# Tail of a feed-forward layer: turns and logits between half product groups, the first expert's low halves on another engine, gates by their own transfer

## Chip, cores and metric

One Trainium2 chip; the kernel runs on 1 of its cores. The metric is the device time of the kernel in microseconds, the median of three timed runs. A profile of one more execution goes with it.

## The reference

Three layers follow one another, all in float32:

```python
mask = q_bucket[:, :, :, None] == k_bucket[:, :, None, :]
scores = np.where(mask, scale * np.matmul(q, k.transpose(0, 1, 3, 2)), -1e9)
attn = np.exp(scores - np.max(scores, axis=-1, keepdims=True))
x = np.matmul(attn / (np.sum(attn, axis=-1, keepdims=True) + 1e-9), v)   # -> (1536, 512)
...
h = x @ w_in                                   # 512 -> 2048
g = (a[0] + a[1]*h + a[2]*h**2 + a[3]*h**3) / (1 + abs(b[0])*abs(h) + abs(b[1])*h**2 + 1e-6)
x = g @ w_out                                  # 2048 -> 512
...
logits = x @ w_gate                            # 8 experts
expert_idx = np.argmax(logits, axis=1)         # one expert for each token
for e in range(E):                             # w1[e]: 512 x 1024, w2[e]: 1024 x 512
    out[mask] = gate_w[mask, None] * (np.maximum(xe @ w1[e], 0.0) @ w2[e])
```

The first layer is attention over 2 x 8 heads of 768 rows, masked by hash buckets. The change concerns the end of the second layer and the third.

## The kernel before

**Products.** Where full precision is wanted, a factor is split in a high part (rounded to TensorE's float32 format) and a low part (what is left), and three matmuls stand for one: high x high, low x high, high x low. ScalarE makes the high halves (a copy), another engine the low halves (a subtraction).

**Feed-forward.** Sixteen steps of 384 tokens and 512 of the 2048 columns. In each step `up` makes four products of h (banks 0 to 2 of PSUM in turn), ScalarE, VectorE and GpSimd make g of each, and `down(s, t)` multiplies four pieces of g with w_out for the token tile t = 0, 1, 2 (banks 4 to 6, twelve matmuls of 512 columns); VectorE adds the bank to y in `y_add`. `down(s, 1)` and `down(s, 2)` stand two steps later, so that at the end of the loop five remain: step 14 (t = 1, 2) and step 15 (t = 0, 1, 2).

**Tail.** y has twelve tiles of 128 tokens, in four chunks of three. For each tile j `turn_y` transposes y into a bank, ScalarE copies it to yt (`y_turned`, two buffers), `logit` multiplies it with w_gate. For each chunk c VectorE's `choose` finds the expert (oh), `ranks` on TensorE counts the tokens ahead, `place` makes the slot numbers, and GpSimd's `route` writes the three tiles of y, with gate and token number as columns 512 and 513, to their slots in HBM (`routed`) by indirect transfers. The order on each engine is written out by hand; each engine works its own list in order and waits on semaphores.

**Table.** From the totals VectorE works out which expert each of 19 tiles of 128 slots belongs to (`tab_ring`, `tab_need`, `tab_rows`, ...), and then increments `table_done`.

**Experts.** For tile t SyncE loads its rows into xg (`rows_in`, two buffers); TensorE has `turn_x`, `mm1` (24 matmuls), `turn_h`, `mm2` (24 matmuls), VectorE `x_in`, `relu`, `h_in`, `y_out`, GpSimd `scatter`. The weights of expert r lie in a ring of two; each matrix comes in two transfers to one staging area, wraw, which is free again when the low halves are made. ScalarE makes sixteen high halves for each expert (`weights_hi`), GpSimd sixteen low halves (`weights_lo`), in this order with the scatters in between:

```python
            for r in range(1, E):
                weights_lo(0, r, range(8))
                weights_lo(1, r, range(8))
                for t in LATE_SCATTERS[r]:
                    scatter(t)
```

with `LATE_SCATTERS = {1: (), 2: (0, 1), 3: (2,), ...}`. In the data of this case tiles 0, 1 and 2 belong to experts 0, 1 and 2, tiles 3 to 10 to expert 3, tiles 11 to 15 to expert 4, and one tile each to the last three. Line numbers are those of the kernel before unless the text says otherwise: L1336 to L1338 down's matmuls, L1347 turn_y, L1357 logit, L726 GpSimd's low halves, L1156 VectorE's copy of the gates, L1433 turn_x, L1447 to L1449 mm1, L1471 to L1473 mm2.

Of the kernel before, what the change touches and what calls it, by code (L numbers as in the profile page):

```python
# [15 lines left out]
P = 128  # L16
# [3 lines left out]
NTOK, DM, DFF = B * S, H * D, 2048  # L20
# [69 lines left out]
def build(nc, q, k, v, proj, w_in, w_out, a, b, w_gate, w1, w2, consts, out):  # L90
    ctx = ExitStack()
    with ctx:
# [16 lines left out]
        def sem(name):  # L109
            return ctx.enter_context(nc.semaphore(name))  # L110
# [120 lines left out]
        put = Map(late)  # L231
        xg = [put(f"xg{i}", [P, ROW], F32) for i in range(2)]
        xth, xtl = [put(x, [P, KD, P], F32R) for x in ("xth", "xtl")]
# [93 lines left out]
        xt_done = sem("xt_done")  # L327
        gi_done = sem("gi_done")
        hs_done = sem("hs_done")
# [34 lines left out]
        def turn_bank(j):  # L364

            return ps[:, 7 * (j % 2), :]

        def logit_bank(c):

            return 1 if c == NCHUNKS - 1 else c + 1  # L370

# [103 lines left out]
        def _(sp):  # L475
# [121 lines left out]
            for c in range(2):  # L597
                load_weights(sp, 0, 1, c)
# [12 lines left out]

# [3 lines left out]
            for t in range(1, NSLOT_TILES):  # L615
                rows_in(t)
            sp.wait_ge(s_xg[0], 16 * (NSLOT_TILES // 2 + 1))
            sp.wait_ge(s_xg[1], 16 * (NSLOT_TILES // 2))


        @block.gpsimd
        def _(pool):
# [136 lines left out]
        def _(act):  # L759
# [140 lines left out]
            for n in range(NSTEP * M4):  # L900
# [6 lines left out]
                if n % (4 * M4) in PIECE_AT and s // 4 + 1 < NQ:  # L907
                    w_piece(s // 4 + 1, PIECE_AT.index(n % (4 * M4)))
            root(NSTEP * M4 - 1)
            g_hi(act, NSTEP * M4 - 2)  # L910
            g_hi(act, NSTEP * M4 - 1)

            act.wait_ge(h_ready, NSTEP * M4)
            act.wait_ge(s_blank_out, 16 * NROUTED // CT)
            weights_hi(0, 0, range(4))
            for j in range(3):
                y_turned(j)
            exps_of(0)
            weights_hi(0, 0, range(4, 8))
            for j in range(3, 6):  # L920
                y_turned(j)
            exps_of(1)
            for j in range(6, 10):
                y_turned(j)
            exps_of(2)
            for j in range(10, 12):
                y_turned(j)
            exps_of(3)
            weights_hi(1, 0, range(8))
            for c in range(2):  # L930
                load_weights(act, 1, 1, c)

# [17 lines left out]
        def _(dve):  # L950
# [154 lines left out]
            def place(c):  # L1105
# [11 lines left out]
            y_add(NSTEP - 2, 1)  # L1117
            y_add(NSTEP - 2, 2)
            y_add(NSTEP - 1, 0)
            place(0)  # L1120
            choose(1)
            y_add(NSTEP - 1, 1)
            place(1)
            choose(2)
            y_add(NSTEP - 1, 2)
            place(2)
# [3 lines left out]
            dve.wait_ge(total_ready, 1)  # L1130
            link(dve.tensor_tensor(cmp[:, :, :], ps[:, 2, 12 * E:13 * E].unsqueeze(2).broadcast_to([P, E, REGION]),
                                   cst[:, C_MULT:C_MULT + E * REGION].rearrange("p (e i) -> p e i", i=REGION), ALU.is_gt))
# [40 lines left out]
            def y_out(t):  # L1173

                dve.wait_ge(mm2_done, t + 1)
                dve.wait_ge(gi_done, t + 1)
# [16 lines left out]
        def _(pe):  # L1193
# [130 lines left out]

            def down(s, t):
# [7 lines left out]
                for m in range(M4):  # L1333
# [5 lines left out]
                mm.then_inc(y_ready, 1)  # L1339

            def turn_y(j):

                pe.wait_ge(y_added, CT * (NSTEP - NCHUNKS) + j + 1)
                if j >= 2:
                    pe.wait_ge(yt_done, j - 1)
                for kt in range(KD):
                    mm = pe.transpose(turn_bank(j)[:, kt * P:(kt + 1) * P], y[:, j, kt:DM:KD], ident)  # L1347
                mm.then_inc(yt_ready, 1)

            def logit(j):  # L1350

                c, i = j // CT, j % CT
                pe.wait_ge(yt_done, j + 1)
                if c == NCHUNKS - 1:
                    pe.wait_ge(slot_done, 2)
                for kt in range(KD):
# [3 lines left out]
            def logits(c):  # L1360

                j = CT * c
                turn_y(j)
                turn_y(j + 1)
                logit(j)
                turn_y(j + 2)
                logit(j + 1)
                logit(j + 2)

# [32 lines left out]
            logits(1)  # L1402
            down(NSTEP - 1, 1)
            ranks(1)
            logits(2)
            turn_y(9)
            down(NSTEP - 1, 2)
            ranks(2)
            turn_y(10)
            logit(9)  # L1410
            logit(10)
            turn_y(11)
            logit(11)
            ranks(3)
            pe.wait_ge(scum_done, NJ)
            pe.matmul(ps[:, 2, 12 * E:13 * E], cst[:, C_ONE:C_ONE + P], scum[:, NJ, :], start=True, stop=True).then_inc(total_ready, 1)

# [10 lines left out]
            def turn_x(t):  # L1428

                pe.wait_ge(s_xg[t % 2], 16 * (t // 2 + 1))  # L1430
# [78 lines left out]
```

## Time and profile before

| | us |
|---|---|
| median of three timed runs | 913.63 (912.94 to 915.4) |
| profiled execution, its time | 916.21 |
| profiled execution, its span | 914.4 |
| TensorE busy | 810.3 (89%) |
| VectorE, ScalarE, GpSimd busy | 586.3, 489.2, 473.7 |
| mean granted TensorE clock | 0.927 |

The span runs from the first to the last instruction. Busy time of TensorE counts an instruction from its start to its modelled end, at either clock; a granted clock of 1.00 is 2.4 GHz and 0.50 is 1.2 GHz. Idle time is put down to what ended it.

### The profile page before, as it was taken

Reading aid. Unit: us, or ns where it says so; the run is one execution under the profiler, and the core shown is the slowest. Engines: PE = TensorE matmul, PEld = TensorE weight load, DVE = VectorE, ACT = ScalarE, POOL = GpSimd, SP = SyncE. Lnnn points to the kernel's source line nnn. Section 1 sums busy time; section 2 is a strip of 40 time slices with the busy share of each in tenths; the row PEclk is TensorE's granted clock in tenths of the full one; section 3 lists DMA queues with packets and bytes.
Section 4 is the critical chain, followed back from the end, with each engine's and each line's share of the span. In section 5 each row is a group of like instructions: output and inputs, shape, how many; then the busy total and the mean of one; then the engine's idle time right before and its main releaser. Section 6 shows DMA issues by size and latency. Waiting matters only on the chain.

```text
span 914.4 us, 12920 instructions
## 1 busy us (share of the span) xinstructions
PE 810.3 (89%) x4222; PEld 711.2 (78%) x4222; DVE 586.3 (64%) x954; ACT 489.2 (53%) x971; POOL 473.7 (52%) x418
## 2 busy tenths in 40 slices
PE   3699999999998899999999979929659799999965
PEld 2589989998977799989999968827547688888844
DVE  2478888888976788787887772474218545445521
ACT  2478877887897787887886773134412000201230
POOL 1223366335365874674774453479788100541696
PEclk9699999999999899999999997659779799999978
DMA  8597877786626509209600402246554200150322
GB/s 186 126 222 175 195 180 175 179 191 145 187 55 218 198 2 344 95 21 340 218 1 7 178 1 70 104 165 227 195 163 157 96 24 24 38 205 13 117 90 103
DMA packets 69103, 124.12 MB, mean 136 GB/s; under 512 B 30670, under 2 KB 33198, under 8 KB 64944
## 3 DMA queue, kind: packets, MB, share of 16 engines
q1 hardware_dynamic: 61248, 89.34, 35.6%
q10 hardware_dynamic: 5312, 27.66, 9.0%
q0 software_dynamic: 2480, 6.31, 1.8%
q8 instruction: 36, 0.59, 0.3%
q14 instruction: 27, 0.22, 0.1%
HBM read 60.21 MB, written 33.45 MB: 102 GB/s over the span
## 4 chain that ended last, share of the span: by engine, by line
PE 76%; POOL 8%; DVE 7%; ACT 4%; issue 2%; SPq 1%; DMA 1%; ACTq 0%; POOLq 0%
POOL split L726 6%; PE ps L1248 6%; PE ps L1337 5%; PE ps L1336 5%; PE ps L1338 5%; PE ps L1322 4%; PE ps L1320 4%; PE ps L1321 4%; PE ps L1471 4%; PE ps L1447 3%; PE ps L1472 3%; PE ps L1473 3%; PE ps L1239 3%; PE ps L1238 3%; PE ps L1260 3%; PE ps L1449 3%
## 5 line engine op out<-in xcount | busy, mean ns | idle before, releaser
L726 POOL TENSOR_TENSOR split<-wraw,split 128x512 fp32r<-128x512 f32 x128 | 159.2, 1281 | 121.3 <-ACT split L874 121.2
L874 ACT ACTIVATE split<-wraw 128x512 fp32r<-128x512 f32 x128 | 67.9, 616 | 220.4 <-PE ps L1449 126.7
L1016 DVE TENSOR_TENSOR ptl<-ps,pth 128x512 fp32r<-128x512 f32 x144 | 98.8, 686 | 36.1 <-ACT pth L812 34.2
L703 POOL TENSOR_TENSOR hw<-hw,ha 128x384 f32<-128x384 f32 x64 | 65.2, 1019 | 78.1 <-ACT hw L886 78.1
L812 ACT ACTIVATE pth<-ps 128x512 fp32r<-128x512 f32 x144 | 86.7, 602 | 31.6 <-PE ps L1248 31.4
L996 DVE TENSOR_REDUCE negmax<-ps 128x1 f32<-128x768 f32 x96 | 91.1, 949 | 13.9 <-PE ps L1239 13.8
L1447 PE MATMUL ps<-split,xth 128*128 (+1 forms) x152 | 66.1, 435 | 34.3 <-POOL split L726 28.0
L1248 PE MATMUL ps<-cst,pr 128*128 128x128 f32 x576 | 88.1, 273 | 1.6 <-ACT pr L803 1.4
L1320 PE MATMUL ps<-xh,wih 128*128 128x384 f32 x256 | 87.1, 340 | 2.0 <-DVE hp L1050 2.0
L803 ACT ACTIVATE pr<-ps,negmax 128x768 f32<-128x768 f32 x96 | 86.8, 904 | 3.2 <-DVE negmax L996 3.2
L1322 PE MATMUL ps<-xh,wil 128*128 128x384 f32 x256 | 86.8, 339 | 0.0
L1321 PE MATMUL ps<-xl,wih 128*128 128x384 f32 x256 | 86.6, 338 | 0.0
L1336 PE MATMUL ps<-woh,gh 128*128 128x512 f32 x192 | 78.4, 408 | 3.0 <-POOL gl L462 3.0
L1162 DVE TENSOR_SCALAR hs<-ps 128x512 f32<-128x512 f32 x38 | 26.2, 691 | 83.5 <-PE ps L1449 83.5
L462 POOL TENSOR_TENSOR gl<-ha,gh 128x384 fp32r<-128x384 f32 x64 | 65.0, 1015 | 27.2 <-ACT gh L456 27.1
L1337 PE MATMUL ps<-wol,gh 128*128 128x512 f32 x192 | 78.6, 409 | 0.0
L1338 PE MATMUL ps<-woh,gl 128*128 128x512 f32 x192 | 78.1, 407 | 0.0
L1248 PEld LDWEIGHTS ps<-cst,pr 128*128 128x128 f32 x576 | 69.8, 140 | 8.9 <-ACT pr L803 2.5
L1260 PE MATMUL ps<-pth,vs 128*128 128x384 f32 x192 | 74.9, 390 | 2.1 <-DVE ptl L1016 0.9
L1238 PE MATMUL ps<-operand 128*128 128x384 f32 x192 | 70.9, 369 | 5.4 <-DMA operand<-mask 5.4
L1471 PE MATMUL ps<-split,hth 128*128 (+1 forms) x152 | 63.5, 418 | 9.2 <-DVE htl L1171 9.2
L1239 PE MATMUL ps<-operand 128*128 128x384 f32 x192 | 66.1, 344 | 0.0
(160 smaller groups left out, 2028.8 us busy)
## 6 DMA issues: line engine op xcount, KB each, us to landing
wraw<-in_moe_w ACTq DMA_DIRECT2D x26, 1024.0 KB, 5.4
routed<-blank SPq DMA_DIRECT2D x32, 771.0 KB, 14.6
operand<-qk_hi SPq DMA_DIRECT2D x16, 384.0 KB, 4.4
operand<-qk_lo SPq DMA_DIRECT2D x32, 192.0 KB, 4.1
operand<-qk_hi SPq DMA_DIRECT2D x32, 192.0 KB, 4.4
operand<-mask SPq DMA_DIRECT2D x16, 384.0 KB, 4.7
wraw<-in_moe_w SPq DMA_DIRECT2D x6, 1024.0 KB, 6.7
xg<-routed SPq DMA_DIRECT2D x19, 257.0 KB, 2.7
```

What stands on the lines that cost most here:

```text
L726: pool.tensor_tensor(split_piece(E_LO[x], r % 2, k), wraw[:, x, i, :], split_piece(E_HI[x], r % 2, k).bitcast(F32), ALU.subtract).then_inc ...
L1016: dve.tensor_tensor(ptl[:, at:at + CW], ps[:, 4 + c % 2, :], pth[:, at:at + CW].bitcast(F32), ALU.subtract).then_inc(ptl_done, 1)
L1238: pe.matmul(bank, operand_of(n, 0)[:, rows], operand_of(n, 2)[:, cols], start=True, stop=False)
L1248: mm = pe.transpose(ps[:, 4 + c % 2, x * P:(x + 1) * P], pr[u % UNITS][:, t, kt * P:(kt + 1) * P], ident)
L1260: pe.matmul(ps[:, 6, 0:HALF], vs[n % 2][:, kt, :], pth[:, cols], start=(kt == 0), stop=False)
L1320: pe.matmul(bank, wh[:, kt, f], xh[bb][:, kt, cols], start=(kt == 0), stop=False)
L1321: pe.matmul(bank, wh[:, kt, f], xl[bb][:, kt, cols], start=False, stop=False)
L1322: mm = pe.matmul(bank, wl[:, kt, f], xh[bb][:, kt, cols], start=False, stop=(kt == KD - 1))
L1336: pe.matmul(ps[:, 4 + t, :], gh[s % 2][:, m, rows], woh[qq % 2][:, m, :], start=(m == 0), stop=False)
L1337: pe.matmul(ps[:, 4 + t, :], gh[s % 2][:, m, rows], wol[qq % 2][:, m, :], start=False, stop=False)
L1338: mm = pe.matmul(ps[:, 4 + t, :], gl[s % 2][:, m, rows], woh[qq % 2][:, m, :], start=False, stop=(m == M4 - 1))
L1471: pe.matmul(ps[:, 2 + t % 2, :], hth[:, kt, :], weights(S_W2H, t, kt), start=(kt == 0), stop=False)
```

## The change

1. **Order on TensorE.** The five last downs are cut in halves of six matmuls, and turns and logits stand between the halves, the logit of a tile one turn behind it. Turns use banks 0 and 1, logits banks 2, 3 and 7. The first turn no longer waits for the last g_done.
2. **Expert 0's weights.** Its low halves are made by VectorE (`first_lo_of`) between `y_add`, `choose` and `place`, where GpSimd made them before; ScalarE makes all sixteen high halves between its copies of yt (before, eight there and eight after the last exps). GpSimd begins expert 1's low halves behind a wait for table_done.
3. **Gates.** xg has 512 columns; gate and token number of a tile go from `routed` straight to gi by a second transfer on the same semaphore. VectorE's copy and the semaphore gi_done are gone.
4. **Expert 1's second matrix** is loaded by SyncE, where ScalarE did it.

```diff
         def logit_bank(c):
-            return 1 if c == NCHUNKS - 1 else c + 1
+            return (2, 3, 7, 2)[c]
...
+            for x in range(2):
+                for c in range(2):
+                    load_weights(sp, x, 1, c)
...
-                    sp.wait_ge(gi_done, t - 1)
...
-                sp.dma_start(xg[t % 2][:, :], rows).then_inc(s_xg[t % 2], 16)
+                sp.dma_start(xg[t % 2][:, :], rows[:, 0:DM]).then_inc(s_xg[t % 2], 16)
+                sp.dma_start(gi[:, t, :], rows[:, DM:ROW]).then_inc(s_xg[t % 2], 16)
...
-            weights_lo(0, 0, range(4))
...
-            route(0)
-            weights_lo(0, 0, range(4, 8))
-            for c in range(1, NCHUNKS):
+            for c in range(NCHUNKS):
                 route(c)
-            weights_lo(1, 0, range(8))
+            pool.wait_ge(table_done, 1)
...
+            def first_lo_of(x, pieces):
...
+                for i in pieces:
+                    dve.wait_ge(e_hi[x], i + 1)
+                    k = piece_place(x, i)
+                    dve.tensor_tensor(split_piece(E_LO[x], 0, k), wraw[:, x, i, :], split_piece(E_HI[x], 0, k).bitcast(F32), ALU.subtract).then_inc(e_lo[x], 1)
...
             y_add(NSTEP - 2, 0)
+            first_lo_of(0, range(0, 4))
+            y_add(NSTEP - 2, 1)
+            first_lo_of(0, range(4, 6))
+            y_add(NSTEP - 2, 2)
+            first_lo_of(0, range(6, 8))
+            first_lo_of(1, range(0, 2))
             choose(0)
...
-                dve.tensor_copy(gi[:, t, :], xg[t % 2][:, DM:ROW]).then_inc(gi_done, 1)
...
-            pe.wait_ge(h_used, NSTEP * M4)
-            pe.wait_ge(g_done, NSTEP * M4)
-            logits(0)
-            down(NSTEP - 2, 1)
-            down(NSTEP - 2, 2)
-            down(NSTEP - 1, 0)
-            ranks(0)
...
+            first, second = slice(0, M4 // 2), slice(M4 // 2, M4)
+            down(NSTEP - 2, 1, first)
+            turn_y(0)
+            down(NSTEP - 2, 1, second)
+            turn_y(1)
+            down(NSTEP - 2, 2, first)
+            logit(0)
+            turn_y(2)
...
```

TensorE at the start of the tail, before. L1347 is the turn of y, L1357 the logit, L1336 the first of the products of `down(14, 1)`:

```order
L1347 MATMUL ps<-cst,y 128x128 x8
L1357 MATMUL ps<-wg,yt_112 128x8 x4
L1347 MATMUL ps<-cst,y 128x128 x4
L1357 MATMUL ps<-wg,yt_113 128x8 x4
L1357 MATMUL ps<-wg,yt_112 128x8 x4
L1336 MATMUL ps<-woh_64,gh_101 128x512
```

The same engine with the change, from the last three of the first six products of `down(14, 2)` on; L1363 is the turn, L1375 the logit, L1350 to L1352 the products:

```order
L1350 MATMUL ps<-woh_64,gh_101 128x512
L1351 MATMUL ps<-wol_65,gh_101 128x512
L1352 MATMUL ps<-woh_64,gl_103 128x512
L1375 MATMUL ps<-wg,yt_112 128x8 x4
L1363 MATMUL ps<-cst,y 128x128 x4
L1350 MATMUL ps<-woh_64,gh_101 128x512
```

Three turns and three logits stood together, and 36 products behind them; now a logit and a turn stand behind every six products.

GpSimd before, from its last low halves of g (L462) on; L732 is the scatter to `routed`, L726 the low halves of weights, L738 the scatter of results:

```order
L462 TENSOR_TENSOR gl_104<-ha_106,gh_102 128x384
L462 TENSOR_TENSOR gl_104<-ha_107,gh_102 128x384
L462 TENSOR_TENSOR gl_104<-ha_108,gh_102 128x384
L726 TENSOR_TENSOR split<-wraw,split 128x512 x4
L732 DMA routed<-y,slot 12288x514 x3
L726 TENSOR_TENSOR split<-wraw,split 128x512 x4
L732 DMA routed<-y,slot 12288x514 x9
L726 TENSOR_TENSOR split<-wraw,split 128x512 x40
```

and with the change (L461 is now the low half of g):

```order
L461 TENSOR_TENSOR gl_104<-ha_106,gh_102 128x384
L461 TENSOR_TENSOR gl_104<-ha_107,gh_102 128x384
L461 TENSOR_TENSOR gl_104<-ha_108,gh_102 128x384
L732 DMA routed<-y,slot 12288x514 x12
L726 TENSOR_TENSOR split<-wraw,split 128x512 x32
L738 DMA out<-yo_157,gi 1536x512
```

Eight low halves stood between the scatters or ahead of them and eight behind them (the first eight of the 40); now the twelve scatters stand together and expert 1's halves come next.

## Rows read from the trace of the kernel before

**Rows 1.** Windows by stage; columns as in its head line, busy time and (instructions).
```profile
core 0: us, PE busy (x) PEld busy (x) DVE busy (x) ACT busy (x) POOL busy (x), PEclk, DMA share, GB/s
541.30:599.20 57.90, 48.63 (x222) 42.72 (x222) 23.26 (x77) 18.53 (x37) 22.63 (x21) 0.69 0.22 78
700.80:722.90 22.10, 15.62 (x63) 12.55 (x62) 15.74 (x12) 0.00 (x0) 10.28 (x9) 0.77 0.55 179
722.90:860.30 137.40, 137.40 (x654) 113.62 (x654) 67.15 (x110) 12.84 (x24) 31.20 (x25) 1.00 0.17 52
860.30:914.40 54.10, 35.19 (x149) 28.10 (x147) 15.81 (x23) 12.71 (x24) 43.51 (x38) 0.84 0.36 126
```

**Rows 2.** Chain of waits, 541 to 640 us: start, us, what.
```profile
556.97 0.43 PE ps L1336
...
565.42 0.23 PE ps L1338
...
566.01 0.56 PE ps L1347 x4
...
571.99 4.61 DVE oh L1092
...
591.32 1.75 PE ps L1357 x16
...
601.71 0.31 DVE te L1142
...
602.26 10.50 DVE tab_ring L1144
...
614.11 19.99 POOL split L726 x16
```

**Rows 3.** Timeline of TensorE: start, us, instruction [idle before <-releaser].
```profile
540.87 0.39 PE L1338 MATMUL ps<-woh,gl 128*128 128x512 f32 x1
...
594.34 1.87 PE L1357 MATMUL ps<-wg,yt 128*128 128x8 f32 x8 [0.69 <-ACT yt L860]
...
608.04 1.12 PE L1433 MATMUL ps<-cst,xg 128*128 128x128 f32 x4 [9.16 <-DMA xg<-routed]
...
646.09 0.79 PE L1447 MATMUL ps<-split,xth 128*128 x1 [7.32 <-POOL split L726]
...
673.00 0.79 PE L1447 MATMUL ps<-split,xth 128*128 x1 [11.64 <-POOL split L726]
```

**Rows 4.** Timeline of VectorE, at the table and at tile 4.
```profile
598.95 0.17 DVE L1112 CAST slot<-slotf 128x3 int32<-128x3 f32 x1
...
613.20 0.17 DVE L1147 TENSOR_SCALAR tab_half<-cend 128x8 int32<-128x8 f32 x1
...
696.01 14.10 DVE L1156 COPY gi<-xg 128x2 f32<-128x2 f32 x1
```

**Rows 5.** Timeline of GpSimd at the same two places.
```profile
602.92 9.79 POOL L726 TENSOR_TENSOR split<-wraw,split 128x512 fp32r<-128x512 f32 x8
...
690.15 19.93 POOL L726 TENSOR_TENSOR split<-wraw,split 128x512 fp32r<-128x512 f32 x16
```

**Rows 6.** Windows, then groups of TensorE lines in the first of them.
```profile
276.00:279.20 3.20, 2.33 (x13) 1.81 (x13) 1.83 (x4) 0.86 (x2) 0.67 (x1) 1.00 0.04 10
...
566.20:569.50 3.30, 3.09 (x27) 2.90 (x26) 0.62 (x4) 1.68 (x3) 1.35 (x2) 1.00 0.00 0
569.70:573.00 3.30, 3.30 (x12) 3.01 (x13) 1.46 (x4) 0.22 (x1) 2.97 (x4) 0.50 0.57 223
...
L1260 PE MATMUL ps<-pth,vs 128*128 128x384 f32 x4 | 1.5, 387 | 0.7 <-DVE ptl L1016 0.7
L1261 PE MATMUL ps<-ptl,vs 128*128 128x384 f32 x4 | 1.3, 336 | 0.0
```

**Rows 7.** Timeline of VectorE near the start.
```profile
11.71 0.96 DVE L962 TENSOR_TENSOR qk_lo<-raw,qk_hi 128x768 fp32r<-128x768 f32 x1
```

**Rows 8.** DMA issues: KB each, median us to landing.
```profile
xg<-routed SPq DMA_DIRECT2D x19, 257.0 KB, 2.7
...
coef<-in_moe_b SPq DMA_DIRECT2D x1, 1.0 KB, 4.1
```

More of the change, by code:

```diff
@@ L231, in build @@
         put = Map(late)
-        xg = [put(f"xg{i}", [P, ROW], F32) for i in range(2)]
+        xg = [put(f"xg{i}", [P, DM], F32) for i in range(2)]
         xth, xtl = [put(x, [P, KD, P], F32R) for x in ("xth", "xtl")]
@@ L596, in _ @@
                     load_weights(sp, x, 0, c)
-            for c in range(2):
-                load_weights(sp, 0, 1, c)
+            for x in range(2):
+                for c in range(2):
+                    load_weights(sp, x, 1, c)
             def rows_in(t):
@@ L616, in _ @@
                 rows_in(t)
-            sp.wait_ge(s_xg[0], 16 * (NSLOT_TILES // 2 + 1))
-            sp.wait_ge(s_xg[1], 16 * (NSLOT_TILES // 2))
+            sp.wait_ge(s_xg[0], 32 * (NSLOT_TILES // 2 + 1))
+            sp.wait_ge(s_xg[1], 32 * (NSLOT_TILES // 2))
         @block.gpsimd
@@ L909, in _ @@
             root(NSTEP * M4 - 1)
+            weights_hi(0, 0, range(0, 2))
             g_hi(act, NSTEP * M4 - 2)
+            weights_hi(0, 0, range(2, 4))
             g_hi(act, NSTEP * M4 - 1)
+            act.wait_ge(s_blank_out, 16 * NROUTED // CT)
+            y_turned(0)
+            weights_hi(0, 0, range(4, 6))
+            y_turned(1)
+            weights_hi(0, 0, range(6, 8))
+            y_turned(2)
             act.wait_ge(h_ready, NSTEP * M4)
[L914 to L917, printed above, removed]
+            weights_hi(1, 0, range(0, 2))
+            y_turned(3)
+            weights_hi(1, 0, range(2, 4))
+            y_turned(4)
             exps_of(0)
-            weights_hi(0, 0, range(4, 8))
-            for j in range(3, 6):
-                y_turned(j)
+            weights_hi(1, 0, range(4, 6))
+            y_turned(5)
+            weights_hi(1, 0, range(6, 8))
+            y_turned(6)
+            y_turned(7)
             exps_of(1)
-            for j in range(6, 10):
+            for j in range(8, 11):
                 y_turned(j)
             exps_of(2)
-            for j in range(10, 12):
-                y_turned(j)
+            y_turned(11)
             exps_of(3)
-            weights_hi(1, 0, range(8))
-            for c in range(2):
-                load_weights(act, 1, 1, c)
             act.wait_ge(table_done, 1)
@@ L1112, in place @@
                 dve.tensor_copy(slot[:, js], slotf[:, js]).then_inc(slot_done, 1)
+            def first_lo_of(x, pieces):
[3 more added lines that the diff above has]
+                    dve.tensor_tensor(split_piece(E_LO[x], 0, k), wraw[:, x, i, :], split_piece(E_HI[x], 0, k).bitcast(F32), ALU.subtract).then_inc(e_lo[x], 1)
             link(dve.tensor_copy(scum[:, 0, :], cst[:, C_BASE:C_BASE + E]))
             y_add(NSTEP - 2, 0)
+            first_lo_of(0, range(0, 4))
[4 more added lines that the diff above has]
+            first_lo_of(1, range(0, 2))
             choose(0)
-            y_add(NSTEP - 2, 1)
-            y_add(NSTEP - 2, 2)
             y_add(NSTEP - 1, 0)
+            first_lo_of(1, range(2, 4))
             place(0)
+            first_lo_of(1, range(4, 6))
+            y_add(NSTEP - 1, 1)
             choose(1)
-            y_add(NSTEP - 1, 1)
+            first_lo_of(1, range(6, 8))
+            y_add(NSTEP - 1, 2)
             place(1)
             choose(2)
-            y_add(NSTEP - 1, 2)
             place(2)
@@ L1323, in up, with down @@
                 mm.then_inc(h_ready, 1)
-            def down(s, t):
+            def down(s, t, part=slice(0, M4)):
                 qq = s // 4
@@ L1332, in down @@
                 rows = slice(t * P, (t + 1) * P)
-                for m in range(M4):
+                for m in range(part.start, part.stop):
                     if t == 0:
@@ L1338, in down @@
                     mm = pe.matmul(ps[:, 4 + t, :], gl[s % 2][:, m, rows], woh[qq % 2][:, m, :], start=False, stop=(m == M4 - 1))
-                mm.then_inc(y_ready, 1)
+                if part.stop == M4:
+                    mm.then_inc(y_ready, 1)
             def turn_y(j):
                 pe.wait_ge(y_added, CT * (NSTEP - NCHUNKS) + j + 1)
+                pe.wait_ge(h_used, NSTEP * M4)
                 if j >= 2:
@@ L1355, in logit @@
                     pe.wait_ge(slot_done, 2)
+                elif c:
+                    pe.wait_ge(g_done, NSTEP * M4)
                 for kt in range(KD):
@@ L1358, in logit @@
                 mm.then_inc(lg_ready, 1)
[L1360 to L1368, printed above, removed]
             def ranks(c):
@@ L1394, in _ @@
             pe.wait_ge(s_wgate, 16)
-            pe.wait_ge(h_used, NSTEP * M4)
-            pe.wait_ge(g_done, NSTEP * M4)
-            logits(0)
-            down(NSTEP - 2, 1)
-            down(NSTEP - 2, 2)
-            down(NSTEP - 1, 0)
-            ranks(0)
-            logits(1)
-            down(NSTEP - 1, 1)
+            first, second = slice(0, M4 // 2), slice(M4 // 2, M4)
[6 more added lines that the diff above has]
+            turn_y(2)
+            down(NSTEP - 2, 2, second)
+            logit(1)
+            turn_y(3)
+            down(NSTEP - 1, 0, first)
+            logit(2)
+            turn_y(4)
+            down(NSTEP - 1, 0, second)
+            logit(3)
+            turn_y(5)
+            down(NSTEP - 1, 1, first)
+            ranks(0)
+            logit(4)
+            turn_y(6)
+            down(NSTEP - 1, 1, second)
+            logit(5)
+            turn_y(7)
+            down(NSTEP - 1, 2, first)
+            logit(6)
+            turn_y(8)
+            down(NSTEP - 1, 2, second)
             ranks(1)
-            logits(2)
+            logit(7)
             turn_y(9)
-            down(NSTEP - 1, 2)
-            ranks(2)
+            logit(8)
             turn_y(10)
             logit(9)
+            turn_y(11)
             logit(10)
-            turn_y(11)
+            ranks(2)
             logit(11)
@@ L1415, in _ @@
             pe.wait_ge(scum_done, NJ)
-            pe.matmul(ps[:, 2, 12 * E:13 * E], cst[:, C_ONE:C_ONE + P], scum[:, NJ, :], start=True, stop=True).then_inc(total_ready, 1)
+            pe.wait_ge(slot_done, 4)
+            pe.matmul(ps[:, 3, 12 * E:13 * E], cst[:, C_ONE:C_ONE + P], scum[:, NJ, :], start=True, stop=True).then_inc(total_ready, 1)
             rings, needs = [0], [8]
```

8 lines of the change are left out of this document (3 added, 5 removed).

## The prediction

> **What bounds the kernel now.** I read the stage table first. From 722.9 to 860.3 us TensorE (PE) is busy throughout at full clock: eleven expert tiles in 137.4 us, 12.5 us each [rows 1]. The 54.1 us behind it hold the last tiles, whose weights are split only when tile 15 has freed its ring slot; both start from the same event, so whatever brings tile 6 forward (it starts at 722.9) brings the end forward by as much. The reader is to see that the places where time can be won lie ahead of 722.9, in three stretches.
>
> First, the tail of the feed-forward, 541.3 to 599.2: PE is called 84% busy, but at a mean granted clock of 0.69 [rows 1]. The chain of waits runs through it: products at 0.43 us each at the lower level and 0.23 us at the upper, turns and logits in blocks, and a VectorE (DVE) instruction on 24 numbers of 4.61 us [rows 2].
>
> Second, from the last slot number to the expert stage. The last cast to slot ends at 599.12 [rows 4]; I call this moment S. DVE's table then stands 10.50 us in a tab_ring instruction on 20 numbers [rows 2], which ends when GpSimd's (POOL) run of eight low halves ends, 602.92 to 612.71 [rows 5]. table_done comes at 613.37 [rows 4], expert 1's low halves start at 614.11 [rows 2].
>
> Third, tile 3 waits 11.64 us and tile 2 waits 7.32 us for POOL's low halves [rows 3]. The chain is POOL's: sixteen halves take 19.99 us [rows 2], then the next expert's. At 696.01 DVE copies two gate columns for 14.10 us, while POOL works from 690.15 to 710.08 [rows 4, 5]; relu, hth and htl of tile 4 stand behind it, and the tile takes 22.1 us instead of 12.5, at a clock of 0.77 [rows 1].
>
> **The tail, part by part.** PE's last product of the loop starts at 540.87 [rows 3], so the tail starts at 541.2. Five down products (60 instructions) at 0.23 make 13.8 us, twelve turns at 0.56 make 6.7, twelve logits at 1.75 / 2 make 10.5 [rows 2], three rank pairs (half a logit's instructions each) 1.3. Now half products stand between a turn and its logit, so ScalarE's (ACT) copies of yt no longer stop PE. I leave 1.0 us of waits: the first turn still needs the last h_used, and logit 0 needs a yt that ACT copies only after its last gh. Sum 33.3, to 574.5. Products end some 7 us before that, and the clock does not last: in the trace it stayed full for 4.1 us of turns and logits behind the products that ended at 565.6, and fell at 569.7 [rows 6]. So I let the last 3 us run at the lower level: 2.5 us more, logit 11 ends at 577.0. From its end (594.34 + 1.87) to S lie 2.9 us in the trace [rows 3, 4], and that chain is unchanged. New S: 579.9, which is **19.2 us earlier**.
>
> What is laid under it: sixteen low halves on DVE. The nearest row of an SBUF subtraction there is 128x768 in 0.96 us [rows 7], so 0.64 each, 10.2 in all. DVE was busy 23.3 us of the 57.9 [rows 1], 4.4 of them the stall; 29 in 38.7 leaves room. I followed the order: ranks 0 is reached by PE at about 559, and choose(0) has made oh by about 556 even with ten halves ahead of it; ranks 1 comes at 568, oh at 565. Without that cover each half that is late would cost 0.64. ACT gets its second eight high halves here too; it was busy 18.5 us of the 57.9 [rows 1], so a few more go into its gaps. POOL has only the twelve scatters.
>
> **The table.** With POOL silent tab_ring should take 0.18 like its neighbours, four more instructions take 0.6, and ACT's first high half 0.74 (613.37 to 614.11) [rows 2, 4]: expert 1's low halves start at S + 4.7, against S + 15.0 now. That is **10.3 us**. If the last scatter holds it, 0.5 less. PE's own road to tile 0 is S + 8.9 for the turn (608.04 [rows 3]), 1.1 for the turn, 1.4 for two copies: S + 11.5. Tile 0's and tile 1's work until the second turn_h took from 614.83 to 638.8 (646.09 less the wait of 7.3 [rows 3]), 23.9 us, so PE is free at S + 35.5, and expert 2's first eight halves are ready at S + 36.7. POOL's chain still sets it, by 1.2 us.
>
> Because PE then waits 1 instead of 7 us, tile 2 starts at full clock: it ran about 12 products at 0.43 instead of 0.23 [rows 2], **2.5 us**. They pass on, since expert 3's halves wait in POOL's queue behind scatter 1, which needs tile 1's second product behind tile 2's first. Bound: nothing to 2.5.
>
> **The gates.** The copy leaves DVE, so tile 4 should take 12.5 instead of 22.1: **9.6 us** [rows 1]. In its place SP issues a second small transfer per tile on the same semaphore, and turn_x waits for both. The bounds are 2.7 us for xg and 4.1 for the 1 KB of coef [rows 8]: landing up to 1.4 us later. For tile 0 that takes the 1.2 us of slack, and I charge 1 us. Later tiles are loaded two ahead, with 25 us (two tiles), at no cost. For x_in the wait for gates has gone; y_out loses one too.
>
> **The second expert's second half** is loaded from SP behind DVE's low halves, done by about 575. Before, ACT issued it at the end. It waited for table_done anyway, so nothing is gained but its landing, which is not on the chain. SP is then free for rows_in before S.
>
> **The sum.** 19.2 + 10.3 + 2.5 + 9.6 - 1.0 = 40.6. The profiled execution took 916.21 us with a span of 914.4; the median of the three timed ones is 913.63. I take the difference from the median: **873 us**.
>
> **A page that speaks against it.** In 276.0 to 279.2 the clock stayed full with eight products of 384 columns and 0.7 us of waits; in 566.2 to 569.5, full of turns and logits only, it was full and then fell to half [rows 6]. The new order has six products of 512 columns in every 2.9 us, the same number of product columns as the first. The Trainium skill, "TensorE: Matmul & The Clock Gate", Part 4, says that a transpose does not count as PE work for the clock gate. By that the turns here would be as good as idle time, and the mix is nearer to a fall than PE's busy time suggests; a fall at the first wait would give rival 1's time. The trace agrees in part: turns and logits together did not hold the clock.
>
> **Rivals.**
> 1. *The clock falls in the mix and stays low.* At 0.5 the products take 0.43, and the trace rose only after long runs of products alone, which the new order doesn't have. The weak place is the wait before logit 0, near 547. From 549 on, 25.5 us of PE work become about 47: S at 600, gain 40.6 - 20 = 20: 893. Falling half way, near 560: S at 591, 884. For it: rows 6 and the wait. Against: the stretch with eight products of 384 kept it in spite of its waits. Chance 0.25.
> 2. *VectorE or the shared port becomes the wait.* The instructions of 4.61 and 10.50 us show that DVE and POOL exclude each other on some SBUF work [rows 2, 5]. DVE's halves now meet POOL's scatters. The table's reduce at 601.71, just behind POOL's scatters and ahead of its long run, took 0.31 us [rows 2], which speaks against it. If each of the last three groups of scatters lost 2 us, S and the table come 6 later: 879. The Trainium skill, "SBUF — State Buffer", section "SBUF: two separate sides", has the port pair as an exclusive lock; by it two-input DVE work waits only on POOL work that reads SBUF. Chance 0.05.
> 3. *The stalls move on.* Another DVE instruction is caught at tile 4, or tiles 0 and 1 end later than POOL, and 8 to 10 us are not won: 882. Against: every DVE instruction left in the expert stage reads PSUM, and the two long ones [rows 4] are those that work from SBUF to SBUF. Chance 0.05.
> 4. *Slower than before: the gate transfer is late for every tile.* It decides once both transfers take more than the 25 us between turn_x(t-2) and turn_x(t); to lose the 40.6 us and 3 more over 17 tiles they would need about 28. The smallest transfers seen took 4.1 [rows 8], so 0.02.
> The forecast has the rest, 0.63.
>
> **How the numbers follow.** The forecast's own range is 868 to 880 (the late clock from 0 to 5, tile 2's clock 0 or 2.5, the transfer 0 to 1.4, the port 0.5, and the spread of the timed runs). Rivals 2 and 3 lie within or next to it, rival 1 from 880 to 894. 867 to 892 leaves out some of each end. About 0.3% is what a measurement of this kernel can tell: all but rival 4 and a little unseen lie well below, so faster 0.97, same 0.01, slower 0.02.
>
> **What would show it.** Right: clock 1.0 from 541 to about 571, last slot near 580, tab_ring at 0.2 us, POOL's first low half at S + 4.7, tile 3 at S + 61, no tile of over 13 us between tile 4 and tile 15. Wrong: 0.43 us products in the tail (rival 1), lows on DVE above 0.7 us or a stretched table (2), any long DVE instruction behind 690 (3), TensorE waiting for gi (4).

## The result, and the profile after

| | before | changed |
|---|---|---|
| median of four timed runs, us | 913.5 (912.94 to 915.4) | 868.45 (865.25 to 870.5) |
| profiled execution, its time and span, us | 916.21, 914.4 | 869.42, 867.3 |
| mean granted clock | 0.927 | 0.956 |

The ratio is 0.95 [0.9466 to 0.9534]: 45 us faster where 40.6 were forecast, 868.45 against 873. Between the two profiled executions the span is 47.1 us shorter; some 1.8 us of that came before the tail, from nothing in the change (see below). Line numbers are now those of the changed kernel: L1350 to L1352 down's products, L1363 the turn, L1375 the logit, L1121 VectorE's low halves, L1461 turn_x, L1475 to L1477 mm1. The runs of the kernel before drifted from 913.5 to 917.73 us between the sets of runs below, so kernels of different sets are compared by their ratio to it.

Windows by stage, for [rows 1] (the tail, the stretch from the last slot number S to tile 3, the stretch of tile 4, the eleven even tiles behind it):

```profile
core 0: us, PE busy (x) PEld busy (x) DVE busy (x) ACT busy (x) POOL busy (x), PEclk, DMA share, GB/s
541.10:577.30 36.20, 34.18 (x216) 31.36 (x216) 27.63 (x90) 18.69 (x37) 11.76 (x12) 0.89 0.54 175
577.30:639.80 62.50, 37.20 (x160) 30.28 (x160) 22.27 (x43) 25.40 (x48) 54.53 (x46) 0.77 0.60 194
666.70:679.10 12.40, 12.40 (x64) 10.47 (x62) 6.07 (x10) 0.00 (x0) 10.68 (x9) 1.00 0.73 215
679.10:814.60 135.50, 135.50 (x661) 114.25 (x661) 65.91 (x100) 13.40 (x26) 31.12 (x25) 1.00 0.19 61
```

The tail is 36 us instead of 58 at a clock of 0.89 instead of 0.69. Tile 4, whose window was 22.1 us at 0.77, is like every other, at 1.00. The eleven tiles behind it take less too, which no step of the prediction has.

The chain of waits through the tail, for [rows 2]:

```profile
544.98 0.59 ACT yt L857
545.61 1.06 PE ps L1375 x8
546.66 0.56 PE ps L1363 x4
547.23 0.23 PE ps L1350
...
568.65 0.79 PE ps L1375 x8
569.44 0.85 PE ps L1363 x4
570.29 1.51 PE ps L1375 x8
...
580.61 0.41 DVE tab_need L1161
581.46 0.64 ACT split L871
582.23 18.54 POOL split L726 x15
```

Products stay at 0.23 us, a logit takes 0.79 and then 1.51: the clock was full up to 569.5 and half from 569.75, 4.2 us behind the last product. What "would show it" named is there: last slot number at 577.27 (S; 580 was forecast), VectorE's low halves at 0.62 to 0.64 us each but for the first four (0.82, beside a low half of g that GpSimd ends at 546.15), tab_ring at 0.18 us, GpSimd's first low half at S + 4.96 and tile 3 at S + 62.55 (S + 61 was forecast), and then, from the timelines of VectorE, GpSimd and TensorE, for [rows 3 to 5]:

```profile
545.23 3.27 DVE L1121 TENSOR_TENSOR split<-wraw,split 128x512 fp32r<-128x512 f32 x4
...
550.83 2.48 DVE L1121 TENSOR_TENSOR split<-wraw,split 128x512 fp32r<-128x512 f32 x4
...
577.10 0.17 DVE L1114 CAST slot<-slotf 128x3 int32<-128x3 f32 x1
...
580.40 0.18 DVE L1160 TENSOR_SCALAR tab_ring<-te 128x20 int32<-128x20 f32 x1
```

```profile
582.23 19.79 POOL L726 TENSOR_TENSOR split<-wraw,split 128x512 fp32r<-128x512 f32 x16 [1.20 <-ACT split L871]
603.97 19.94 POOL L726 TENSOR_TENSOR split<-wraw,split 128x512 fp32r<-128x512 f32 x16 [1.95 <-ACT split L871]
624.08 1.01 POOL L738 DMA_INDIRECT out<-yo,gi  x1 [0.16 <-issue]
628.89 0.98 POOL L738 DMA_INDIRECT out<-yo,gi  x1 [3.80 <-DVE yo L1193]
```

```profile
586.24 1.13 PE L1461 MATMUL ps<-cst,xg 128*128 128x128 f32 x4 [9.21 <-DMA gi<-routed]
...
614.10 0.79 PE L1475 MATMUL ps<-split,xth 128*128 x1 [2.24 <-POOL split L726]
639.82 0.79 PE L1475 MATMUL ps<-split,xth 128*128 x1 [11.64 <-POOL split L726]
```

The 47.1 us by the moments of the two traces: S 21.85; S to GpSimd's first low half 10.0 (15.0 to 4.96); from there to tile 3's mm1 1.3 more; mm1 of tile 3 to mm1 of tile 6 49.87 to 39.23, so 10.6; mm1 of tile 6 to that of tile 17 138.24 to 135.60, so 2.6; 0.6 behind it.

Of the first 21.85 us, 1.77 were there before the tail began: the last product of `up` starts at 538.16 before and at 536.39 with the change. In both executions the clock fell to half at 303.3 us, early in the feed-forward, where the two kernels are alike. It rose again at 310.2 before and at 306.7 with the change; 3.4 us less at half speed are 1.7 us. The fourteen profiles of this document have that last product between 535.2 and 538.2, with the kernel before at the late end. So the tail itself gave 20.1 us, and 45.3 us of the 47.1 are the change's, which is what the medians say.

### The profile page after: what moved, and what is told of

It reads as the page before. It is cut to its first block, busy times and chain, and to the rows that moved or that the text cites. A ratio compares the mean times of both kernels' runs of the same rounds, so it can differ in the third digit from the quotient of the medians.

```text
span 867.3 us, 12938 instructions
## 1 busy us (share of the span) xinstructions
PE 784.7 (90%) x4222; PEld 694.3 (80%) x4222; DVE 563.0 (65%) x951; ACT 489.0 (56%) x971; POOL 454.0 (52%) x402
## 4 chain that ended last, share of the span: by engine, by line
PE 78%; POOL 9%; ACT 4%; DVE 3%; issue 2%; SPq 2%; DMA 1%; ACTq 0%; POOLq 0%
POOL split L726 7%; PE ps L1262 6%; PE ps L1351 5%; PE ps L1352 5%; PE ps L1350 5%; PE ps L1334 5%; PE ps L1336 5%; PE ps L1335 5%; PE ps L1475 4%; PE ps L1274 4%; PE ps L1476 4%; PE ps L1477 4%; PE ps L1253 4%; PE ps L1252 4%; PE ps L1501 3%; PE ps L1499 3%
## 5 line engine op out<-in xcount | busy, mean ns | idle before, releaser
L726 POOL TENSOR_TENSOR split<-wraw,split 128x512 fp32r<-128x512 f32 x112 | 139.4, 1283 | 109.7 <-ACT split L871 109.7
L1475 PE MATMUL ps<-split,xth 128*128 (+1 forms) x152 | 65.0, 427 | 25.4 <-POOL split L726 23.2
L1336 PE MATMUL ps<-xh,wil 128*128 128x384 f32 x256 | 86.3, 337 | 0.0
L461 POOL TENSOR_TENSOR gl<-ha,gh 128x384 fp32r<-128x384 f32 x64 | 65.0, 1015 | 27.0 <-ACT gh L455 26.9
L1350 PE MATMUL ps<-woh,gh 128*128 128x512 f32 x192 | 75.9, 395 | 3.0 <-POOL gl L461 3.0
L1352 PE MATMUL ps<-woh,gl 128*128 128x512 f32 x192 | 75.9, 395 | 0.0
L1351 PE MATMUL ps<-wol,gh 128*128 128x512 f32 x192 | 75.8, 395 | 0.0
L1193 DVE TENSOR_SCALAR yo<-ps,gi 128x512 f32<-128x512 f32 x19 | 14.3, 751 | 77.7 <-PE ps L1501 77.7
```

The source lines that it names most:

```text
L726: pool.tensor_tensor(split_piece(E_LO[x], r % 2, k), wraw[:, x, i, :], split_piece(E_HI[x], r % 2, k).bitcast(F32), ALU.subtract).then_inc ...
L1336: mm = pe.matmul(bank, wl[:, kt, f], xh[bb][:, kt, cols], start=False, stop=(kt == KD - 1))
L1475: pe.matmul(ps[:, c, :], xth[:, kt, :], weights(S_W1H, t, k), start=(kt == 0), stop=False)
```

## Experiments

**Each part alone.** `e1_lows_alone` is the kernel before with part 2: sixteen low halves on VectorE between y_add, choose and place, all high halves in the tail, GpSimd waits for table_done. `e6_order_alone` is part 1: the changed kernel with the other parts undone but for SyncE's load and the place of ScalarE's high halves. These stand in the tail in both kernels, so what they are worth may be in both gains. `e2_gates_alone` is part 3 put into the kernel before.

The cores of the three edits, in that order (the second against the changed kernel):

```diff
-            weights_lo(0, 0, range(4))
...
-            weights_lo(1, 0, range(8))
+            pool.wait_ge(table_done, 1)
...
+            first_lo_of(0, range(4))
             choose(0)
+            first_lo_of(0, range(4, 8))
```

```diff
+            weights_lo(0, 0, range(4))
...
-            pool.wait_ge(table_done, 1)
+            weights_lo(1, 0, range(8))
...
-            first_lo_of(0, range(0, 4))
```

```diff
+                sp.dma_start(gi[:, t, :], rows[:, DM:ROW]).then_inc(s_xg[t % 2], 16)
...
-                dve.tensor_copy(gi[:, t, :], xg[t % 2][:, DM:ROW]).then_inc(gi_done, 1)
```

> The kernel before with the second part alone: VectorE makes the first expert's sixteen low halves, GpSimd has only scatters until table_done; TensorE's order is that of before. Theory (GpSimd's run of halves shuts VectorE's SBUF-to-SBUF work out): the instruction of 4.6 us in the second choose and the 10.5 us of tab_ring both fall to 0.2, so 913.5 - 4.4 - 10.3 = 899 us (896 to 902), S earlier by about 4.4. Rival (these instructions are slow of their own, for their integer output or their place): tab_ring stays near 10 us, 908 to 914 us.

> The kernel before with the third part alone (gates by their own transfer); xg keeps its size of 514 columns, so that every buffer keeps its address. Theory (the 14.1 us copy at tile 4 was the stall): tile 4 takes 12.6 us instead of 22.1 and nothing else changes: 913.5 - 9.6 = 904 us (902 to 906), products of the expert stage still at 0.2335 us. Rival (another instruction is caught there, or the second transfer costs time for each tile): 909 us or more.

> The new order on TensorE and ScalarE alone: GpSimd makes the first expert's low halves where it made them before, VectorE copies the gates, xg is as before. Theory (the parts add): S is some 20 us earlier, the stalls of 10.5 us in the table and of about 14 us in the gates' copy stay: 892 us (888 to 896). Rival (the parts need each other: the halves now meet the choose steps in a fuller tail): S only 10 to 15 us earlier, 898 us or more.

| one set, kernel before 914.82 | us | ratio | won |
|---|---|---|---|
| lows alone | 894.43 | 0.9791 [0.9758 to 0.9824] | 19 |
| gates alone | 905.66 | 0.9901 [0.9877 to 0.9925] | 9 |
| order alone | 894.25 | 0.979 [0.9757 to 0.9823] | 19 |

The three gains add up to 47, where the whole change has 43 to 49: within the some 5 us that the three intervals leave together, nothing large is won twice or lost between them. Gates alone takes tile 4 to 12.57 us and leaves the rest. Order alone brings S to 580.33 and leaves both stalls of VectorE, which its timeline shows as

```profile
583.46 10.49 DVE L1157 TENSOR_SCALAR tab_ring<-te 128x20 int32<-128x20 f32 x1
...
673.92 14.11 DVE L1169 COPY gi<-xg 128x2 f32<-128x2 f32 x1
```

A third stall is left in its tail, 5.89 us for three instructions on 8 numbers beside four of GpSimd's low halves. From the last product of `up` to S it takes 44.1 us, where the whole change takes 40.9.

Lows alone won 4 to 5 us more than I had expected. tab_ring took 0.17 and GpSimd began at S + 4.96, as it should, but S itself came 11.2 us earlier, where 4.4 were expected. Of these, 1.7 us are again from ahead of the tail. Windows of the same stretches, before and then lows alone:

```profile
559.00:573.00 14.00, 13.79 (x73) 12.13 (x72) 3.97 (x10) 1.91 (x4) 4.51 (x5) 0.87 0.15 58
573.00:587.90 14.90, 14.27 (x60) 12.10 (x60) 8.02 (x25) 2.39 (x5) 6.45 (x6) 0.61 0.36 124
```

```profile
559.00:573.00 14.00, 13.79 (x86) 12.11 (x84) 5.14 (x22) 4.40 (x9) 3.08 (x3) 1.00 0.39 132
573.00:587.90 14.90, 12.47 (x87) 11.56 (x86) 10.44 (x40) 5.47 (x12) 5.95 (x6) 0.89 0.34 104
```

TensorE was as busy in the first stretch, but at full clock, and so ahead. A block of turns, logits and ranks without products lies there in both, from 565.65 before and from 563.65 with lows alone. Before, the clock fell 3.9 us into it; with lows alone products followed after 5.0 us and it held, as it did through 5.4 us in the second stretch. The kernels with the new order of TensorE show the same scatter. Their block behind the last product is the same work in eight of them, yet the clock fell 4.1 to 4.2 us into it in three (the changed kernel among them), after 5.0 and 5.6 us in two (scatter later, both) and after 7.9 to 8.1 us in three (copy back, load by ScalarE, load later). Why it held longer in some isn't shown. So some of these 4 to 5 us may not belong to part 2, and S by itself differs by up to 2.1 us between kernels whose tails are alike.

**What holds VectorE.** `e12_no_table_wait` is the changed kernel with GpSimd free to begin expert 1's low halves before the table is made.

```diff
-            pool.wait_ge(table_done, 1)
...
-            act.wait_ge(table_done, 1)
             for r in range(1, E):
+                if r == 2:
+                    act.wait_ge(table_done, 1)
```

> The changed kernel in which expert 1's high and low halves do not wait for table_done: GpSimd goes on with the sixteen halves right behind the last scatter. Theory (GpSimd's unbroken run shuts out VectorE): a table instruction takes 10 to 20 us, tile 0's first product starts 5 to 15 us later than 589, and the kernel takes 873 to 881 us although expert 1's halves start 1 to 2 us earlier. Rival (no exclusion): the halves start 1 us earlier and the kernel takes 867 us.

879.01 us, ratio 0.9605 [0.9575 to 0.9636]: some 10 us lost again. VectorE and GpSimd:

```profile
579.40 20.26 DVE L1160 TENSOR_SCALAR tab_ring<-te 128x20 int32<-128x20 f32 x1
```

```profile
580.07 19.56 POOL L726 TENSOR_TENSOR split<-wraw,split 128x512 fp32r<-128x512 f32 x16
610.13 10.05 POOL L726 TENSOR_TENSOR split<-wraw,split 128x512 fp32r<-128x512 f32 x8 [10.50 <-ACT split L870]
```

An instruction on 20 numbers is held until 599.66; GpSimd's sixteen end at 599.63. So the stall follows the length of GpSimd's run: eight halves 10.50 us [rows 2, 5], sixteen 20.26. (By the profile the held instruction starts some 0.67 us ahead of the run in both; why is not shown, and a scatter of GpSimd's ends just ahead of the run.) GpSimd began at S + 3.8 instead of S + 4.96, and then waited 10.50 for ScalarE, which had waited for the table.

Not every instruction is held to the end of a run. In the kernel before, this copy of the gates stands in the middle of sixteen halves (614.11 to 634.09):

```profile
625.34 1.26 DVE L1156 COPY gi<-xg 128x2 f32<-128x2 f32 x1
```

It ends with the tenth of them, at 626.60. Each copy of two columns that is stretched in these traces ends with one of GpSimd's instructions: many with the next to end, after at most 1.3 us, and a few only with the last (14.1 us at tile 4). What decides between the two isn't shown. The Trainium skill, "SBUF — State Buffer", section "SBUF: two separate sides", has the shared port pair as an exclusive lock that is held for the whole instruction. The short stalls agree with that; the long ones show VectorE kept out over a whole run of instructions.

**The copy of the gates put back** in the changed kernel, with the buffers behind xg at the changed kernel's distance from a multiple of 128 bytes.

```diff
-        xg = [put(f"xg{i}", [P, DM], F32) for i in range(2)]
+        xg = [put(f"xg{i}", [P, ROW], F32) for i in range(2)]
+        put.at += 64
...
-                sp.dma_start(gi[:, t, :], rows[:, DM:ROW]).then_inc(s_xg[t % 2], 16)
+                dve.tensor_copy(gi[:, t, :], xg[t % 2][:, DM:ROW]).then_inc(gi_done, 1)
```

> The changed kernel with only the gates' part undone: one transfer of 514 columns and VectorE's copy to gi, with a gap so that all later buffers keep the addresses of the changed kernel. Theory (the copy is caught by GpSimd's run): one copy near tile 4 takes over 10 us and the kernel 868.45 + 9.8 = 878 us (874 to 880). Rival (the copy was caught by chance of position and now passes): all copies at 0.2 to 2 us, 868 to 870 us.

880.88 us, ratio 0.9628 [0.9607 to 0.9649]: just above the expected 874 to 880, 12 us of the gain lost by the ratios. Two copies are held until one of GpSimd's runs ends (618.43 and 657.80); five others that fall into a run end with the next of its instructions, after 0.44 to 1.13 us:

```profile
618.43 2.09 DVE L1174 COPY gi<-xg 128x2 f32<-128x2 f32 x1
...
657.80 14.12 DVE L1174 COPY gi<-xg 128x2 f32<-128x2 f32 x1
```

The tile in which it stands 14.12 us takes 22.02, the others 12.53. By that 9.5 us are the stall and 2.2 eleven slower tiles.

**The pitch of a tile.** The changed kernel's 12.33 us for a tile against 12.57 needed an explanation. xg with 512 columns also moves every buffer behind it by 64 bytes, so two kernels move them back without another change.

```diff
         xg = [put(f"xg{i}", [P, ...], F32) for i in range(2)]
+        put.at += 64
```

> The kernel before with nothing changed but an unused gap of 64 bytes behind xg, so that xth, xtl, hth, htl and hs start at multiples of 128 bytes as they do in the changed kernel (in the kernel before they start 64 bytes past one). Seen in the changed kernel: products of the expert stage every 0.2285 us instead of 0.2335, a tile every 12.33 us instead of 12.57. Theory (the address does it): 913.5 - 14 tiles on the path x 0.24 = 910.1 us (909 to 911), tile every 12.33 us. Rival (it comes from something else in the change, as VectorE's or SyncE's work beside it): 913.5, tile every 12.57 us.

> The changed kernel with the opposite shift: 64 unused bytes behind xg put the same buffers 64 bytes past a multiple of 128. Theory (address): 868.45 + 3.4 = 872 us, a tile every 12.57 us. Rival: 868.5 us, a tile every 12.33 us.

| kernel | columns of xg | buffers behind it, from a multiple of 128 bytes of their area | tile, us | time, us; ratio |
|---|---|---|---|---|
| before | 514 | 64 | 12.57 | |
| gates alone | 514 | 64 | 12.57 | 905.66 |
| before, shifted | 514 | 0 | 12.53 | 915.61; 1.0002 [0.9988 to 1.0017] |
| copy back | 514 | 0 | 12.53 | 880.88 |
| changed, shifted | 512 | 64 | 12.56 | 872.93; 0.9525 [0.9511 to 0.954] |
| changed (another set) | 512 | 0 | 12.33 | 868.45; 0.95 |

The eleven tiles by windows, changed and shifted, then before and shifted:

```profile
665.70:803.80 138.10, 138.10 (x661) 114.43 (x661) 65.90 (x100) 12.84 (x24) 37.45 (x31) 1.00 0.26 79
```

```profile
721.40:859.20 137.80, 137.80 (x663) 114.67 (x662) 67.80 (x111) 13.49 (x26) 31.17 (x25) 1.00 0.17 52
```

Moving the buffers by 64 bytes takes the faster pitch away from the changed kernel, but doesn't give it to the one before. So this distance alone is no explanation. The two kernels at distance 0 that are slow have 514 columns (with the second xg then 32 bytes further off) and the copy of the gates; which of these has a part in it, and how, stays open. All of it is in the products: 48 of them at 0.2285 us instead of 0.2335 are 0.24 us, the whole difference.

**The second matrix of expert 1** loaded again by ScalarE at the end of the tail.

```diff
-            for x in range(2):
-                for c in range(2):
-                    load_weights(sp, x, 1, c)
+            for c in range(2):
+                load_weights(sp, 0, 1, c)
...
             exps_of(3)
+            for c in range(2):
+                load_weights(act, 1, 1, c)
```

> The changed kernel with the fourth part undone: ScalarE issues the two transfers of expert 1's second matrix behind the last exps. Theory (off the chain, all landed before ScalarE needs them): 868.5 us, within 1. Rival (the second transfer lands behind ScalarE's eighth high half and GpSimd's chain waits): 870 to 873 us.

872.11 us, ratio 0.9527 [0.9511 to 0.9544], which is nearer to the rival; the interval overlaps that of the changed kernel, so the times alone don't decide. The traces decide. SyncE's load, TensorE's first turn_x and GpSimd:

```profile
584.16 0.33 SPq L608 DMA_DIRECT2D xg<-routed  x1
```

```profile
589.82 1.13 PE L1462 MATMUL ps<-cst,xg 128*128 128x128 f32 x4 [16.09 <-DMA gi<-routed]
```

```profile
600.58 10.00 POOL L725 TENSOR_TENSOR split<-wraw,split 128x512 fp32r<-128x512 f32 x8 [2.17 <-ACT split L870]
614.84 10.03 POOL L725 TENSOR_TENSOR split<-wraw,split 128x512 fp32r<-128x512 f32 x8 [4.25 <-ACT split L870]
```

The load of tile 0's rows is issued 5.8 us behind GpSimd's last scatter of y, where it was 2.2, and its data are there 5.7 us later instead of 3.0. In those stretches two transfers of 1 MB issued from 571.54 on and one issued at 583.68 are under way beside the scatters and the load; between the load's issue and its data the DMA engines are busy to 0.89, where it was 0.34. The first turn_x comes at S + 15.9 instead of S + 9.0, and GpSimd waits 2.17 and 4.25 us instead of 1.95 once. Tile 3 starts at S + 65.0 instead of S + 62.55. So part 4 is worth some 2.4 us of the chain, which I had put at nothing. Other kernels with SyncE's load have tile 3 between S + 61.1 (copy back) and S + 62.7 (whole groups), so it is 2.3 to 3.9 us by these traces. Lows alone, which also has ScalarE's late load, shows the same delay: rows issued at S + 9.8, turn_x at S + 13.2. That the transfers slow each other is read from these moments, not tried by itself.

**Coarser mixing.** Whole groups of twelve products, with two turns and two logits between them.

```diff
-            down(NSTEP - 2, 1, first)
+            down(NSTEP - 2, 1)
             turn_y(0)
-            down(NSTEP - 2, 1, second)
             turn_y(1)
...
```

> The changed kernel with whole groups of twelve products and two turns and two logits between them, where it has halves of six and one turn and one logit; all else is as changed. The same work in the same stretch, mixed twice as coarsely. Theory (TensorE stays busy and the clock holds as long as products come back within some 3 us): clock 1.00 from 541 to about 569, 868.5 us (867 to 871). Rival (the clock falls in a stretch with turns and logits only and does not come back): products at 0.43 us in the tail, S near 590, 878 to 890 us.

871.4 us, ratio 0.9499 [0.9475 to 0.9523], and S at 576.41: no different from the changed kernel within the intervals. The stretches without products are 2.6 to 3.1 us long between groups, and the clock held through all of them. It fell at 565.5 (569 was expected), 3.8 us behind the last product, and was half from there:

```profile
565.70:572.70 7.00, 7.00 (x35) 7.00 (x36) 2.62 (x15) 1.30 (x3) 1.92 (x2) 0.50 0.51 199
```

**Two waits that are left.** Tile 3 still waits 11.64 us for GpSimd. `e7_scatter_later` moves scatter 1, for which GpSimd waited 3.80 us, behind the next sixteen halves. `e8_load_later` lets ScalarE's queue issue the last load behind the next first halves. `e9_both` has both.

```diff
e7: -        LATE_SCATTERS = {1: (), 2: (0, 1), 3: (2,), ...}
e7: +        LATE_SCATTERS = {1: (), 2: (0,), 3: (1, 2), ...}
e8: +                    if x == 0 and r > 1:
e8: +                        load_weights(act, 1, r, 1)
...
e8: -                        for c in range(2):
e8: +                        for c in range(2 - x):
```

> The changed kernel with tile 1's scatter behind expert 3's halves instead of expert 2's. In the changed kernel GpSimd ends expert 2's halves at 623.9 us, then waits for this scatter until 628.9 and starts expert 3's at 629.9; ScalarE's high halves for them begin at 624.9. Theory (the scatter holds the chain to tile 3): expert 3's halves start at 625.7, tile 3 at 635.7 instead of 639.8, and everything behind follows: 864.3 us (863 to 866). Rival (given back before the end, as the last tiles hang on something else): 868 us.

> The changed kernel with the last of an expert's four weight transfers issued by ScalarE behind the next expert's first eight high halves instead of ahead of them, since it waits for GpSimd's last low half and the high halves don't. Theory: the 1.95 us between GpSimd's runs of expert 1 and 2 go, and 0.6 us at the last expert: 866 us (865 to 867.5). Rival (the high halves of the second matrix then come late, as their transfer lands later): 868 to 871 us.

> Both of the two edits before in one kernel. Theory (they add): 862 us (860 to 864). Rival: no better than the better one alone, 864 to 866 us.

| one set, kernel before 917.73 | us | ratio |
|---|---|---|
| scatter later | 868.15 | 0.9466 [0.9444 to 0.9489] |
| load later | 867.98 | 0.947 [0.945 to 0.9491] |
| both | 864.64 | 0.9425 [0.9404 to 0.9445] |
| whole groups (for comparison) | 871.4 | 0.9499 [0.9475 to 0.9523] |

GpSimd with both, and TensorE at tile 3 there:

```profile
581.59 39.82 POOL L726 TENSOR_TENSOR split<-wraw,split 128x512 fp32r<-128x512 f32 x32 [1.20 <-ACT split L871]
621.55 1.01 POOL L738 DMA_INDIRECT out<-yo,gi  x1
```

```profile
632.57 0.79 PE L1477 MATMUL ps<-split,xth 128*128 x1 [8.45 <-POOL split L726]
```

Thirty-two halves run without a break and one scatter stands before expert 3's: they start at S + 45.96 instead of S + 52.59, and tile 3 at S + 55.96 instead of S + 62.55. Each edit alone has an interval that touches the changed kernel's; both together is clear of it, 7 us by the ratios. The set's kernel before is 4 us slower than in the first set, so the ratios are to be held against the expectations: 864.3, 866 and 862 of 913.5 us are 0.946, 0.948 and 0.944, and all three are met. Both together is the fastest version that was run. That GpSimd's chain sets the time of the first tiles is shown by it: 6.6 us off the one are 6.6 us off the other, of which some 1.2 are the clock at tile 2, which held here.

## Why the prediction was right, step by step

- **The tail: 19.2 us forecast, 21.85 found, 20.1 of them its own.** Right in kind: no product at the lower level, two waits of TensorE at its start (0.27 and 0.51, 1.0 was charged), the clock lost 4.2 us behind the last product as [rows 6] had it, and 2.91 us from the last logit to S. The 1.8 us from ahead of the tail are the clock at 303 us. Most of what the tail gave beyond the forecast is the logits: I took half of 1.75 us for each, and most took 0.79, nearly 1 us less in all. The lower clock cost what it was given (4.9 us of work at half, so 2.4). That it fell after 4.2 us and not after 8, as in three other kernels with this tail, is chance as far as is known.
- **VectorE has room for the low halves.** Right: 10.9 us for sixteen against 10.2 (the first four took 0.82 each, above the 0.7 named as a sign of rival 2, which came to 0.7 us in all), no late one on the chain, the table at full pace.
- **The table: 10.3 forecast, 10.0 found** (S + 4.96 for S + 4.7). The mechanism is shown by lows alone and by the run without the wait.
- **Tile 2 at full clock: 2.5 forecast, about 1.3 found** in the changed kernel's trace. Tile 2 waited 2.24 us instead of 7.32, but TensorE still ran at the lower level from 613.8 to 617.3. That isn't so in every trace: with waits of 2.03 and 2.09 (changed and shifted, copy back) the clock held, and tile 2's mm1 to tile 3's took 24.49 and 24.43 us, where it was 26.91 before and 25.72 here. There the term is 2.4 to 2.5 as forecast, and tile 3 comes at S + 61.4 and S + 61.1. The size was right; that the clock would hold was not certain, and with a wait of 2.42 (whole groups) it fell too. The mechanism that passes it on is the one named: scatter 1, for which GpSimd stands 3.80 us; the run with that scatter moved shows it.
- **The gates' copy: 9.6 forecast, 9.8 found** at tile 4 (0.2 of it from the faster products), 9 us by itself and 9.5 when put back.
- **The second transfer: 1.0 charged, nothing found.** Both transfers land in 2.6 us by the profile's list of DMA issues, and turn_x of tile 0 comes at S + 8.97, where [rows 3, 4] have S + 8.92. The 4.1 us of coef, taken as the bound, are of a single transfer at the start of the kernel.
- **Expert 1's second matrix: nothing forecast, 2.4 us or more found.** The step that failed is "its landing, which is not on the chain". Without part 4 its landing wasn't late, but the transfer itself stood beside the last scatters and held the first rows back. In the sum it is hidden: S + 8.97 for turn_x would have been later without it.
- **Not forecast at all: 2.6 us** from the faster products of the even tiles.

Rival 1 (the clock falls in the mix) didn't come in any of the runs with that order, nor with pauses of up to 3.1 us between groups of products. The Trainium skill's rule that a transpose does not count for the clock gate ("TensorE: Matmul & The Clock Gate", Part 4) is not refuted by that: the clock fell where turns and logits stood alone, 3.8 to 8.1 us behind the last product, but in the mix there was no fall. Rivals 2 to 4 are out: no long instruction of VectorE is left, no tile from 4 to 15 takes above 12.4 us, and TensorE waits for gi only at tile 0. The median lies in the forecast's own range by its lower end, because the small terms that were wrong mostly had the same sign: logits 1.0 us, the transfer 1.0, the faster products 2.6 and more, against 1.2 the other way at tile 2. The faster products are luck: no step had them, and their cause is open.

## What to carry to other kernels

Look for instructions on a few numbers that take many microseconds: here three of them (4.6, 10.5 and 14.1 us) ended with a run of another engine, and two of them alone were worth 20 of the 45 us. Take such an instruction off the engine, or put the other engine's run behind it. Short latency-bound pieces go between halves of a long product stream, and it doesn't matter much how finely. A transfer of a megabyte that isn't urgent should be started well ahead of the small one on which everything waits, not beside it.

## What the hardware showed that was not expected

- VectorE was held for sixteen instructions of GpSimd in a row (20.26 us); one of them takes 1.24 (19.79 / 16). Other instructions that met such a run were let in at the end of the next one (1.26 us), and nothing here tells them apart.
- The same matmuls took 0.2285 or 0.2335 us each at full clock, and 64 bytes in the place of their operands were enough to change it in one of two kernels.
- The same turns and logits behind the last product were left at full clock for 4.2 us in the changed kernel and for 8.1 us in the kernel with the later load.
